# Token places of all experts from products with the running counts, a later second weights load, and one fp16 column of token numbers

## The reference

```python
for idx in order:                      # argsort(-logits)
    tok, e = (int(idx) // E, int(idx) % E)
    if assigned[tok] >= 0 or counts[e] >= cap:
        continue
    assigned[tok] = e
    counts[e] += 1
for e in range(E):
    mask = assigned == e
    h = np.maximum(x[mask] @ w1[e], 0.0)     # 512 -> 1024
    out[mask] = h @ w2[e]                    # 1024 -> 512
```

## Time and profile before

| | us |
|---|---|
| median of 3 runs | 855.26 (854.28 to 857.5) |
| the profiled execution | 852.95 |
| its span, first to last instruction | 851.2 |
| TensorE busy | 793.9 (93%) |
| VectorE busy | 523.0 (61%) |
| ScalarE busy | 274.1 (32%) |
| GpSimd busy | 99.7 (12%) |
| mean granted TensorE clock, share of 2.4 GHz | 0.974 |

### The profile page before, as it was taken

How to read it: one execution, slowest core, us unless ns; L and a number is a source line. 1 busy time by engine, 2 the same in 40 slices (tenths; PEclk the granted TensorE clock), 3 DMA queues, 4 the chain that set the end, 5 groups by cost and what they waited for, 6 DMA issues and landing times.

```text
span 851.2 us, 14868 instructions
## 1 busy us (share of the span) xinstructions
PE 793.9 (93%) x5504; PEld 649.9 (76%) x5504; DVE 523.0 (61%) x1241; ACT 274.1 (32%) x592; POOL 99.7 (12%) x144
## 2 busy tenths in 40 slices
PE   6999999999999943999999998999999999999996
PEld 4677777676767633899899997998888788878885
DVE  5887788877888689596797784264333433333331
ACT  3566666666666510122211211232110311130111
POOL 4111221312223301010011010000000100010001
PEclk9999999999999975799999999999999999999999
DMA  6114415053250206065155146640000100010001
GB/s 131 39 38 109 97 38 126 20 124 84 52 126 10 78 20 222 2 224 195 42 211 213 60 176 223 259 163 1 1 1 0 50 0 0 0 49 0 0 0 49
DMA packets 74602, 68.78 MB, mean 81 GB/s; under 512 B 52288, under 2 KB 60480, under 8 KB 73536
## 3 DMA queue, kind: packets, MB, share of 16 engines
q1 hardware_dynamic: 70976, 60.82, 23.8%
q0 software_dynamic: 2240, 7.34, 2.4%
q10 hardware_dynamic: 1344, 0.04, 0.1%
HBM read 61.90 MB, written 6.29 MB: 80 GB/s over the span
## 4 chain that ended last, share of the span: by engine, by line
PE 82%; DVE 9%; DMA 5%; issue 2%; ACT 1%; POOL 1%; SPq 0%; ACTq 0%; DVEq 0%; POOLq 0%
PE pt_ps L1326 15%; PE score_ps L1309 15%; PE pt_ps L1232 9%; PE pt_ps L1134 8%; PE pt_ps L1242 6%; PE score_ps L1106 4%; PE pv_ps L1106 4%; PE score_ps L1090 4%; PE score_ps L1091 4%; DMA area<-x_rows,ids_now 4%; PE work_ps L1179 2%; DVE area L955 2%; DVE area L898 1%; PE work_ps L1062 1%; PE score_ps L1062 1%
## 5 line engine op out<-in xcount | busy, mean ns | idle before, releaser
L1326 PE MATMUL pt_ps<-y_s,w_in_s 128*128 128x512 f32 x576 | 137.8, 390 | 2.7 <-DVE y_s L1017 2.0
L1309 PE MATMUL score_ps<-w_out_s,gate_s 128*128 128x512 f32 x576 | 137.4, 389 | 0.0
L1326 PEld LDWEIGHTS pt_ps<-y_s,w_in_s 128*128 128x128 f32 x576 | 107.9, 188 | 26.1 <-DVE y_s L1017 2.8
L1309 PEld LDWEIGHTS score_ps<-w_out_s,gate_s 128*128 128x128 f32 x576 | 108.1, 188 | 22.4
L1035 DVE TENSOR_TENSOR gate<-pt_ps,sig 128x512 f32<-128x512 f32 x48 | 33.2, 692 | 146.4 <-ACT sig L597 146.4
L483 ACT ACTIVATE att_area<-att_area 128x768 f32<-128x768 f32 x96 | 90.0, 937 | 87.9 <-DVE att_area L793 87.8
L793 DVE TENSOR_SCALAR_CACHE_REDUCE att_area<-score_ps 128x768 f32<-128x768 f32 x96 | 91.7, 955 | 21.0 <-PE score_ps L1091 19.6
L1232 PE MATMUL pt_ps<-area,experts_w 128*128 128x192 f32 x512 | 98.7, 341 | 2.9 <-ACT area L557 2.9
L597 ACT ACTIVATE sig<-pt_ps 128x512 f32<-128x512 f32 x48 | 28.7, 598 | 210.5 <-PE pt_ps L1326 210.5
L1242 PE MATMUL pt_ps<-area,experts_w 128*128 128x192 f32 x512 | 89.0, 329 | 1.3 <-ACT area L561 1.3
L1232 PEld LDWEIGHTS pt_ps<-area,experts_w 128*128 128x128 f32 x512 | 84.1, 194 | 3.9 <-ACT area L557 3.9
(11 more groups left out here) (190 smaller groups left out, 935.7 us busy)
## 6 DMA issues: line engine op xcount, KB each, us to landing
experts_w<-in_moe_w SPq DMA_DIRECT2D x16, 2048.0 KB, 9.1
experts_w<-in_k SPq DMA_DIRECT2D x16, 384.0 KB, 4.8
experts_w<-in_q SPq DMA_DIRECT2D x16, 384.0 KB, 5.5
experts_w<-in_moe_w_in SPq DMA_DIRECT2D x8, 512.0 KB, 4.8
w_out_raw<-in_moe_w_out SPq DMA_DIRECT2D x4, 1024.0 KB, 8.9
att_area<-in_v SPq DMA_DIRECT2D x16, 192.0 KB, 2.3
x_rows<-att_area SPq DMA_DIRECT2D x8, 384.0 KB, 3.5
area<-x_rows,ids_now POOLq DMA_INDIRECT x16, 5.4
```

What stands on the lines that cost most here:

```text
L1309: done = nc.tensor.matmul(out_ps[m], gate_s[:, fo % RING_S, a, m * P:(m + 1) * P], w_out_s[:, fo, b, :], start=(fo == 0 and a + b == 0), s ...
L1326: done = nc.tensor.matmul(layer_ps[f % 2][:, 0:GT], w_in_s[:, a, w_cols], y_s[:, c, b, :], start=(c == 0 and a + b == 0), stop=(c == DC - ...
```

## The change

Seven edits belong together.

- `count(r)` is now 13 matmuls with the whole `assigned` (bf16) as moving operand: 12 with `ones`, each shifted by one tile further and so of 96, 88, ... 8 columns, and one of 96 columns with `upto`. They sum in PSUM to `places_ps`: for every expert and token the token's place, and in a thirteenth column group the expert's total count (`count_ps`).
- `prefix`, `mine`, `mine_pairs`, `mine_before` and `got_sum` are gone. `mark(r)` multiplies `places_ps` with the mask of the chosen expert and sums: that is `slot`.
- `filled` is copied from the total at the start of `find_best(r)`, no longer added up. `find_best(0)` skips the closing of full experts.
- Token numbers are one fp16 column (`token_id`), so `token_of_slot` has matmuls of 1 column, and `find_ids` is a copy. Its matmuls wait for each one-hot tile, not for all 12, and run tile by tile.
- In round 1, find_slots(0) and find_ids(0) come ahead of find_best(1) on VectorE, and `token_of_slot(0)` ahead of `row_of_best(1)` on TensorE.
- SyncE issues an expert's `w2` load only when both row gathers of that expert have landed.
- The clearing of half of `one_hot` moves from VectorE to GpSimd, and `load_rows` waits without the extra semaphore increment of `hold`.

```diff
-        upto = sb("upto", [P, P])
+        upto = sb("upto", [P, P], bf16)
         after = sb("after", [P, P], bf16)
         ones = sb("ones", [P, P], bf16)
         e_rank = sb("e_rank", [P, E])
-        earlier = sb("earlier", [P, NT, NT])
-        slot_row = sb("slot_row", [P, CAP], bf16)
-        id_parts = sb("id_parts", [P, NT, 3], bf16)
+        slot_row = sb("slot_row", [P, CAP], f16)
+        token_id = sb("token_id", [P, NT, 1], f16)
...
-        count_ps = pv_ps[:, 64:64 + E]
-
-        perm_ps = pv_ps[:, 128:128 + 3 * 2].rearrange("p (m c) -> p m c", c=3)
-        prefix_ps = pv_ps[:, 192:192 + NT]
+
+        places_ps = pv_ps[:, 256:256 + (NT + 1) * E].rearrange("p (t e) -> p t e", e=E)
+        count_ps = places_ps[:, NT, :]
+
+        perm_ps = pv_ps[:, 128:128 + 2]
...
                 if r >= 2:
                     sp.wait_ge(s_e, ESTEPS * (r - 2) + ESTEPS)
+                for m in range(2):
+                    sp.wait_ge(s_rows[m], 16 * r + 16)
                 sp.dma_start(w2_sb[i], w2_rows[bass.ds(e, 1)].rearrange("e p j d -> p (e j) d")).then_inc(s_w2[i], 16)
...
-                parts = id_parts[:, :, :].rearrange("p (b t) c -> p b t c", b=B)
-                step(nc.gpsimd.iota(parts[:, :, :, 0], pattern=[[0, B], [0, T]], base=0, channel_multiplier=1, **small))
-                step(nc.gpsimd.iota(parts[:, :, :, 1], pattern=[[0, B], [1, T]], base=0, channel_multiplier=0, **small))
-                step(nc.gpsimd.iota(parts[:, :, :, 2], pattern=[[1, B], [0, T]], base=0, channel_multiplier=0, **small))
+                by_batch = token_id[:, :, 0].rearrange("p (b t) -> p b t", b=B)
+                step(nc.gpsimd.iota(by_batch, pattern=[[S, B], [1, T]], base=0, channel_multiplier=T, **small))
...
+            pool.wait_ge(s_best, 1)
+            nc.gpsimd.memset(one_hot[:, :, CAP:PT], 0.0).then_inc(s_cleared, 1)
+
             def load_rows(r):
 
                 if r == 0:
                     pool.wait_ge(s_xw, 16 * PAIRS)
-                hold(s_ids, r + 1)
+                pool.wait_ge(s_ids, r + 1)
...
             def find_best(r):
 
-                step(nc.vector.tensor_scalar(penalty[:, :], filled[:, :], float(CAP), CLOSED, ALU.is_ge, ALU.mult))
-                step(nc.vector.tensor_tensor(open_logits[:, :, :], logits[:, :, :], over_tiles(penalty[:, :]), ALU.add))
-                nc.vector.tensor_reduce(best[:, :], open_logits[:, :, :], X, ALU.max).then_inc(s_best, 1)
+                if r:
+                    step(nc.vector.tensor_copy(filled[:, :], count_ps))
+                    step(nc.vector.tensor_scalar(penalty[:, :], filled[:, :], float(CAP), CLOSED, ALU.is_ge, ALU.mult))
+                    step(nc.vector.tensor_tensor(open_logits[:, :, :], logits[:, :, :], over_tiles(penalty[:, :]), ALU.add))
+                nc.vector.tensor_reduce(best[:, :], (open_logits if r else logits)[:, :, :], X, ALU.max).then_inc(s_best, 1)
...
-            def count_got(r, taken):
-
-                step(nc.vector.tensor_reduce(penalty[:, :], taken.rearrange("p t e -> p e t"), X, ALU.add))
-                nc.vector.tensor_copy(got_sum[:, :], penalty[:, :]).then_inc(s_got, 1)
-                step(nc.vector.tensor_tensor(assigned[:, :, :], assigned[:, :, :], taken, ALU.add))
+            def assign(r, taken):
+
+                if r >= 1:
+                    dve.wait_ge(s_count, r)
+                nc.vector.tensor_tensor(assigned[:, :, :], assigned[:, :, :], taken, ALU.add).then_inc(s_assigned, 1)
 
             def round_end(r):
 
@@ -914,21 +912,14 @@
                 step(nc.vector.tensor_reduce(worst[:, :], load[:, :, :], X, ALU.max))
                 step(nc.vector.scalar_tensor_tensor(now[:, :], worst[:, :], float(CAP), pending[:, :], ALU.is_le, ALU.mult))
                 step(nc.vector.tensor_tensor(got[:, :, :], wants[:, :, :], over_experts(now[:, :]), ALU.mult))
-                count_got(r, got[:, :, :])
+                assign(r, got[:, :, :])
                 step(nc.vector.tensor_tensor(pending[:, :], pending[:, :], now[:, :], ALU.subtract))
+
+            def pick(r):
+
+                i = r % 2
                 dve.wait_ge(s_count, r + 1)
-                step(nc.vector.tensor_tensor(filled[:, :], filled[:, :], count_ps, ALU.add))
-
-            def last_round_end(r):
-
-                count_got(r, wants[:, :, :])
-                dve.wait_ge(s_count, r + 1)
-                step(nc.vector.tensor_tensor(filled[:, :], filled[:, :], count_ps, ALU.add))
-
-            def pick(r):
-
-                i = r % 2
-                step(nc.vector.scalar_tensor_tensor(left_full[:, :], filled[:, :], float(CAP), left[:, :],
+                step(nc.vector.scalar_tensor_tensor(left_full[:, :], count_ps, float(CAP), left[:, :],
...
-                nc.vector.scalar_tensor_tensor(left[:, :], left[:, :], chosen[:, 0:1], left[:, :],
-                                               ALU.not_equal, ALU.mult)
-                step(nc.vector.tensor_reduce(mine[:, :], choice_key[:, :, :], X, ALU.add))
-                step(nc.vector.tensor_tensor(mine_pairs, mine[:, :].unsqueeze(1).broadcast_to([P, NT, NT]),
-                                             earlier[:, :, :], ALU.mult))
-                nc.vector.tensor_reduce(mine_before[:, :], mine_pairs, X, ALU.add).then_inc(s_mine, 1)
+                step(nc.vector.tensor_tensor(choice_key[:, :, :], places_ps[:, 0:NT, :], choice_key[:, :, :], ALU.mult))
+                step(nc.vector.tensor_reduce(slot[:, :], choice_key[:, :, :], X, ALU.add))
 
             def find_slots(r):
 
-                dve.wait_ge(s_prefix, r + 1)
-                step(nc.vector.tensor_tensor(slot[:, :], prefix_ps, mine[:, :], ALU.mult))
                 for j in range(NT):
                     nc.vector.tensor_scalar(one_hot[:, j, CAP * (r % 2):CAP * (r % 2 + 1)], slot_row[:, :], slot[:, j:j + 1], None,
                                             ALU.is_equal).then_inc(s_hot, 1)
+                step(nc.vector.scalar_tensor_tensor(left[:, :], left[:, :], chosen[:, 0:1], left[:, :],
+                                                    ALU.not_equal, ALU.mult))
 
             def find_ids(r):
 
                 dve.wait_ge(s_perm, r + 1)
-                step(nc.vector.tensor_scalar(id_mid[:, :], perm_ps[:, :, 0], float(T), None, ALU.mult))
-                step(nc.vector.tensor_tensor(id_mid[:, :], id_mid[:, :], perm_ps[:, :, 1], ALU.add))
                 if r >= 2:
                     for k in range(2):
                         dve.wait_ge(s_rows[k], 16 * (r - 1))
-                nc.vector.scalar_tensor_tensor(ids_now[:, r % 2, :], perm_ps[:, :, 2], float(S), id_mid[:, :],
-                                               ALU.mult, ALU.add).then_inc(s_ids, 1)
-                nc.vector.scalar_tensor_tensor(ids[:, id_cols(r)], perm_ps[:, :, 2], float(S), id_mid[:, :],
-                                               ALU.mult, ALU.add).then_inc(s_kept, 1)
+                nc.vector.tensor_copy(ids_now[:, r % 2, :], perm_ps).then_inc(s_ids, 1)
+                nc.vector.tensor_copy(ids[:, id_cols(r)], perm_ps).then_inc(s_kept, 1)
 
             find_best(0)
             find_wants(0)
-            nc.vector.memset(one_hot[:, :, CAP:PT], 0.0)
...
                     mark(0)
+                    find_slots(0)
+                    find_ids(0)
                     find_best(1)
-                    find_slots(0)
                     find_wants(1)
                 else:
                     find_best(r)
@@ -988,13 +971,14 @@
                     find_slots(r - 1)
                 if r < E - 1:
                     compare(r, 0)
-                find_ids(r - 1)
+                if r > 1:
+                    find_ids(r - 1)
                 for i in range(1, NT if r < E - 1 else 1):
                     compare(r, i)
                 if r < E - 1:
                     round_end(r)
                 else:
-                    last_round_end(r)
+                    assign(r, wants[:, :, :])
...
             def count(r):
-                pe.wait_ge(s_got, r + 1)
-                nc.tensor.matmul(count_ps, ones[:, :], got_sum[:, :], start=True, stop=True).then_inc(s_count, 1)
-
-            def prefix(r):
-
-                pe.wait_ge(s_mine, r + 1)
-                nc.tensor.matmul(prefix_ps, upto[:, :], mine[:, :], start=True, stop=False)
-                nc.tensor.matmul(prefix_ps, ones_f[:, :], mine_before[:, :], start=False, stop=True).then_inc(s_prefix, 1)
+
+                pe.wait_ge(s_assigned, r + 1)
+                for s in range(1, NT + 1):
+                    nc.tensor.matmul(places_ps[:, s:NT + 1, :], ones[:, :], assigned[:, 0:NT + 1 - s, :],
+                                     start=(s == 1), stop=False, skip_group_check=True)
+                nc.tensor.matmul(places_ps[:, 0:NT, :], upto[:, :], assigned[:, :, :],
+                                 start=False, stop=True, skip_group_check=True).then_inc(s_count, 1)
 
             def token_of_slot(r):
 
```

(24 more changed lines are left out.)

27 lines of the change are left out of this document (10 added, 17 removed).

## The result

| | before | after |
|---|---|---|
| median, same chip | 854.77 us (854.27 to 857.5) | 842.54 us (841.36 to 842.99) |
| the profiled execution | 852.95 | 842.99 |
| its span | 851.2 | 841.2 |
| share of TensorE, VectorE, DMA in the chain that ended last | 82, 9, 5% | 89, 5, 1% |

A forecast was written before the change was run, and what follows sets the result against it. TensorE's own work was taken to bound the full rounds, small VectorE chains counting only in rounds 0, 1 and 7. Terms 3.8 + 3.9 + 2.2 = 9.9 us off the 855.26 us median gave 845.4 us, range 842.0 to 850.3.

The forecast's parts named there:

- Term 1: Rounds 0 and 1: earlier ids and gather, clearing off VectorE, first rows turned 3.75 us sooner; 3.8 us gained.
- Term 2: The five full rounds, 2 to 6: 0.68 us less per round on TensorE plus 0.5 of row waits; 3.9 us gained.
- (b): Full rounds: the prefix products' 0.36 us of TensorE's time all goes, per round.
- (c): Full rounds: the first comparison is done before TensorE wants its rank, so a 0.26 us wait goes per round.
- The waits for rows: Full rounds: TensorE's waits for gathered rows, 0.5 us in all, go because ids come earlier and no w2 load competes.
- (a): Full rounds, the count: best comes 0.06 us earlier per round; 0.34 us of added matmuls vanish in TensorE's wait for it.
- Term 3: Round 7: second output block 0.62 us earlier, gather issued 1.05 us earlier and landing in 4.8 us; 2.2 us gained.
- The w2 loads: Issued behind the row gathers, they cost nothing; closest in round 7, landed by 539 us and needed near 543.
- A dear count: Rival: each count matmul takes 0.08 us, gain 5.3 us, 850.0; chance 0.09 (gain over 4.3) or 0.08 (under), shared with late w2.
- a chain of counts: Rival: each count matmul waits for the one before, 3.0 us a count, 21 us lost, 866 us; chance 0.04.
- a harmful wait of SyncE: Rival: w2 4 us late in round 7, with old gather landings; 850.3 us; chance 0.09 or 0.08, shared with dear count.
- The clock: Rival: in round 1 full clock comes at the old time and comparisons run late; gain 7.1 us, 848.2; chance 0.13.

The follow-up runs named there:

- experiment 1: The kernel before, with SyncE issuing an expert's second weights only when its two row gathers have landed; 848.51 us, ratio 0.9917.
- experiment 2: The changed kernel with the second weights issued at once, as early as before; 849.19 us, ratio 0.9939.
- experiment 8: The changed kernel with best logits made ahead of marks, slots and ids in round 1, its row turned ahead of the token products; 839.56 us.
- experiment 4: The changed kernel with two unused fp32 products put back between an expert's first and second output block in rounds 2 to 7; 843.06 us.
- experiment 5: The changed kernel with six unused VectorE additions ahead of the first comparison of rounds 2 to 6, so TensorE waits for it; 847.05 us.
- experiment 6: The changed kernel with the thirteen count products issued twice; 845.99 us, ratio 0.9871.
- experiment 10: experiment 8's kernel with best also ahead of the pick in rounds 2 to 6, and a seventh rank product ahead of the first hidden block; 834.44 us.

## Why the prediction came out too small

The direction was right, and of the signs named most came: the first ids at 328.07 where 327.9 stood, the rows turned at 338.4, a count of 0.41 us, no wait for the comparison. Not so the rounds, 30.06 us where 30.3 to 30.5 stood. What failed is the sizing of the second and third term, 1.5 and 1.3 us too small: idle times and single gaps were taken for what a wait or a product costs, and a landing of 4.8 us was taken where 3.2 to 3.4 came. The first term was 0.3 us too large, and its reason was only half the story.

- **Term 1 (3.8, measured 3.54)** held in size, and so did what it named as late next, the comparisons behind the row of best. Wrong is that it took the earlier ids for the source of the gain: experiment 1 gets 3.2 us at the same place by the later load alone, experiment 2 turns them just as early without it, and experiment 8 gets 2.6 more by putting best first again.
- **Term 2 (3.9, measured 5.41)** failed in four numbers. (b) The prefix was read as the 0.36 us between two starts; the output block behind it also ran 0.09 us longer, and what went is 0.45 (experiment 4): 0.45 us over five rounds. (c) The comparison's wait was read as its idle time, 0.26; its distance is 0.40 (experiment 5 prices such a wait at 0.14 above its idle time), and 24 products of one column take 0.02 less: 0.8 us. The waits for rows, 0.5 shown, cost 1.2 by the starts behind them: 0.7 us. Against these stands (a): from the start of the add to VectorE's first step with the count it was 0.95 us where the sum had 0.86, so best came 0.03 later instead of 0.06 earlier, 0.45 us less. Nor do the added matmuls vanish in the wait for best, as the prediction puts it: they stand ahead of best, experiment 6 pays a second set in full, and the first is paid for by the reduction and the cast that went. 0.45 + 0.8 + 0.7 - 0.45 = 1.5 us.
- **Term 3 (2.2, measured 3.51)** failed where a landing of 4.8 us was taken; it was 3.2 to 3.4, below the least row of before (4.2), which had been taken while weights were loaded. So no wait was left: 2.23 us from the end of the output blocks, where the sum had 1.6, and 0.40 more because eight transposes behind a wait take 2.00 us to the next product and without one 1.60. The prefix with its wait gave 0.76 instead of 0.69, the first output block was 0.03 us late instead of 0.07, and the later prefix gave 0.1 more than the count took.
- **The w2 loads** cost nothing, as the prediction had it, and no expert_out waited for them. But the prediction gave their later issue only the waits for rows and a part of term 3, and it is where about half of the gain comes from: with them issued at once the change is worth 5.7 us by the medians (854.91 to 849.19).
- **The rivals.** A dear count, a chain of counts and a harmful wait of SyncE are out (0.41 us, no wait). The clock came back 46.3 us after attention's end instead of 50.0, 7.9 us behind the first turned rows where it had been 8.1. That it moves with the work is not shown beyond this pair: over the twelve profiles the full clock came 4.9 to 8.1 us behind the first turned rows, 6.6 in the second profile of the kernel before. By my estimate 3.2 us of half clock are worth 1.6, so round 1 of a single profile can be off by that much. Of the clock in round 7 the prediction said nothing, though TensorE's wait for the rows there was on the chain.
- **Not run by themselves** were the fp16 column of token numbers, the matmuls that wait tile by tile, and `load_rows` without `hold`. What they are worth is open.

## What to carry to other kernels

Measure a wait or an inserted product on TensorE by the distance between starts on both sides, with and without it: the idle time shown is short by 0.14 us here, and what stands behind it can be slower for a few tenths. A gather whose ids come late landed sooner here with the DMA engines empty (3.2 to 3.4 us against 5.5 to 5.9 in round 7); a load that nobody needs for 20 us can wait for it, and a wait of SyncE is all that it takes. When an edit makes one of two things in a row early, look whether the other is now the late one: here best, not the ids, was worth being first.

## What was not expected of the hardware

- The granted clock behind nearly the same wait of TensorE, 2.06, 2.06 and 1.96 us, differed from run to run: full (before), 0.50 for 3.4 us (before once more), 0.50 for 6.8 us (experiment 2). The same wait costs 2.6 to 5.4 us.
- In round 0 the twelve transposes of the row took 1.50 us in most profiles, and 2.50 and 2.67 at a granted clock of 0.50 in experiments 4 and 10, from the same code and data. The start of attention alone put two profiles of the kernel before 1.9 us apart.
- GpSimd's clearing of 2304 fp16 columns took 2.02 us against 1.02 on VectorE, where it runs as 1152 words of 32 bits, and a VectorE conversion beside it took 0.63 us instead of 0.19.
- The two gathers of the second-last expert's 192 rows landed 3.2 to 3.4 us after issue with the DMA engines nearly empty and 5.5 to 5.9 us beside weights; those of the first expert took 6.1 to 7.4 us beside weights.
